# First unit of an attention and two-MLP kernel in two passes of 256 tokens, begun after two groups, on one core

## The reference, cut to what matters

```python
# attention: batch 4, heads 8, sequence 768, head size 48; y goes to x (3072 tokens x 384)
for t in range(S):
    cur = einsum('bhd,bhe->bhde', u * k_t, v_t)
    y[:, :, t] = einsum('bhd,bhde->bhe', r_t, state + cur)
    state = w_t[..., None] * state + einsum('bhd,bhe->bhde', k_t, v_t)
# first MLP, F1 = 768
h = maximum(maximum(x @ w1, x @ w2), x @ w3)
x = h @ w_out
# second MLP, F2 = 1024
h = x @ w_in;  e = exp(h - max(h));  sm = e / (sum(e) + 1e-9)
solu = h * sm
out = ((solu - mean) / sqrt(var + 1e-6) * g_ln) @ w_out2
```

## Time and profile before

| | |
|---|---|
| time, median of 3 runs (lowest, highest) | 776.88 us (776.53, 777.39) |
| the profiled execution: own time | 776.59 us |
| its span, first to last instruction | 774.8 us |
| TensorE busy (matmuls), weight loads | 727.5 us, 604.1 us |
| VectorE busy | 494.7 us |
| ScalarE, GpSimd busy | 296.4 us, 72.9 us |

### The profile page before, as it was taken

How to read it: one execution, slowest core, us unless ns; L and a number is a source line. 1 busy time by engine, 2 the same in 40 slices (tenths; PEclk the granted TensorE clock), 3 DMA queues, 4 the chain that set the end, 5 groups by cost and what they waited for, 6 DMA issues and landing times.

```text
span 774.8 us, 21949 instructions
## 1 busy us (share of the span) xinstructions
PE 727.5 (94%) x9280; PEld 604.1 (78%) x9280; DVE 494.7 (64%) x944; ACT 296.4 (38%) x698; POOL 72.9 (9%) x178
## 2 busy tenths in 40 slices
PE   4776999999999999999999999999999999999987
PEld 3666778778887778888878888877988877888776
DVE  5998666698455688566589566578665568222381
ACT  4434432674313445132447123336233236211260
POOL 2222301201011101011010011010110100000000
PEclk9956899999999999999999999999999999999999
DMA  7345523155222045420134511216611004400043
GB/s 243 114 129 172 178 87 107 32 152 177 89 79 78 5 126 178 128 78 20 60 109 148 178 51 43 64 42 186 186 45 40 2 7 135 130 10 1 1 136 121
DMA packets 56706, 74.92 MB, mean 97 GB/s; under 512 B 8224, under 2 KB 43296, under 8 KB 56608
## 3 DMA queue, kind: packets, MB, share of 16 engines
q1 hardware_dynamic: 56192, 73.44, 30.0%
q10 hardware_dynamic: 416, 0.08, 0.1%
HBM read 48.58 MB, written 22.54 MB: 92 GB/s over the span
## 4 chain that ended last, share of the span: by engine, by line
PE 78%; DVE 9%; issue 3%; DMA 3%; SPq 2%; ACT 1%; DVEq 0%; ACTq 0%
PE ps L608 17%; PE ps L609 15%; PE ps L610 15%; PE ps L667 14%; PE ps L564 10%; PE ps L585 3%; PE ps L603 3%; DVE z_blocks L869 2%; DVE rk_sb L804 2%; PE ps L594 1%; DMA z_turning<-z_blocks 1%; DMA zT<-z_turning 1%; DVE e_sb L909 1%; DVE neg_max L903 1%; DVE scoresT L825 1%
## 5 line engine op out<-in xcount | busy, mean ns | idle before, releaser
L667 PE MATMUL ps<-w_moe_out,zT 128*128 128x384 f32 x384 | 132.9, 499 | 8.5 <-ACT out_sb L782 4.8
L804 DVE TENSOR_TENSOR rk_sb<-rk_sb,decay 112x512 f32<-112x512 f32 x144 | 97.6, 698 | 54.4 <-PE ps L564 53.6
L608 PE MATMUL ps<-xT,w_moe 128*128 128x512 f32 x324 | 131.0, 404 | 0.3 <-issue 0.3
L667 PEld LDWEIGHTS ps<-w_moe_out,zT 128*128 128x128 f32 x384 | 118.5, 315 | 15.3 <-issue 6.0
L609 PE MATMUL ps<-xT,w_moe 128*128 128x512 f32 x324 | 126.9, 392 | 0.0
L610 PE MATMUL ps<-xT,w_moe 128*128 128x512 f32 x324 | 126.7, 391 | 0.0
L564 PEld LDWEIGHTS ps<-rk_sb 48*64 48x64 f32 x4224 | 86.0, 148 | 50.7 <-issue 34.2
L564 PE MATMUL ps<-rk_sb 48*64 48x32 f32 (+1 forms) x4224 | 98.2, 233 | 20.4 <-DVE rk_sb L804 16.9
L709 ACT COPY scoresT<-ps 16x128 f32<-16x128 f32 (+2 forms) x168 | 55.8, 333 | 87.5 <-PE ps L564 78.5
L752 ACT CAST h_x<-e_sb 128x512 fp32r<-128x512 f32 x36 | 22.4, 621 | 173.9 <-DVE e_sb L888 173.9
L832 DVE COPY_PREDICATED scoresT<-level_m,ps 64x256 f32<-64x256 uint32 x144 | 76.6, 532 | 4.0 <-PE ps L564 1.4
(11 more groups left out here) (78 smaller groups left out, 953.8 us busy)
## 6 DMA issues: line engine op xcount, KB each, us to landing
rk_sb<-in_rk SPq DMA_DIRECT2D x24, 512.0 KB, 4.2
z_turning<-z_blocks SPq DMA_DIRECT2D x24, 512.0 KB, 3.2
zT<-z_turning SPq DMA_DIRECT2D x96, 128.0 KB, 2.9
w_sb<-in_w SPq DMA_DIRECT2D x24, 224.0 KB, 4.0
k_turning<-k_blocks SPq DMA_DIRECT2D x20, 256.0 KB, 2.3
k_tok<-k_turning SPq DMA_DIRECT2D x80, 64.0 KB, 2.2
v_sb<-in_v SPq DMA_DIRECT2D x24, 192.0 KB, 4.2
out<-out_sb SPq DMA_DIRECT2D x24, 192.0 KB, 2.1
```

The source lines that it names most:

```text
L608: nc.tensor.matmul(o, a[0], b[0], start=first, stop=False)
L667: last = nc.tensor.matmul(ps[:, OUT, 0:DM], zT[:, t % 2, :, c], w_moe2_out[:, c, :], start=(c == 0), stop=(c == J2 - 1))
L804: nc.vector.tensor_tensor(both, both, by, ALU.mult).then_inc(scaled, 1)
```

## The change

- The `u` and `d` tasks of unit 0 are done in two passes of 256 tokens (`PASSES`, `tokens`), the first when groups 0 and 1 are done. Words `u`, `d` of the list are pass 0 and `U`, `D` pass 1 of that unit. Every `u` and `d` of both passes has as many matmuls as before, with 256 columns in place of 512. All other units are one pass.
- For groups 0 and 1 (`first`) VectorE masks all 128 tokens of a slot in one operation, on 128 partitions in place of twice 64. The late half's scores then lie in the columns of the early half, and `mix` makes y in two halves, with 24 matmuls on 64 rows of scores in place of 8, after which it needs no state product. The fourth pair of heads is written into its rows of `xT` by matmuls with `v_first` (a copy of v's pieces between zeros, a new DMA), so `y_last` and the six DMAs fall away for these two groups. GpSimd clears the part of `scoresT` afterwards; VectorE's memset at the start falls away.
- For groups 0 and 1 k is turned by four TensorE transposes into bank 7 with an identity (a new DMA on ScalarE's queue) and copied by ScalarE into `k_tok`, in place of VectorE's transpose and the two DMA steps.
- For groups 0 to 3 (`ZERO_GROUPS`) the state products are left out, since the state is zero, and ScalarE copies the update into `state` in place of VectorE's two operations.
- The four strings are written anew. In the new list the first `u` stands behind 22 slots (all of groups 0 and 1, five of group 2, one of group 3), two `M` and chunks 0 to 10. The second unit's first `u` stands in both lists behind the same work: all of unit 0, `M` 0 to 7, slots up to the sixth of group 8 and the second of group 9.

```diff
+PASSES = [B // 2, B // 2] + [B] * (UNITS - 1)
+P0 = [sum(PASSES[:n]) for n in range(len(PASSES) + 1)]
+ZERO_GROUPS = B
+FIRST_GROUPS = B // 2
...
-    v q 3 4 3 4 3 p b4 b5 4 z z M q p v z 4 a5"""
+    z 0 1 a2 0 1 0 z z z 1 z M q v 1 b2 2 2 1 2 z 2 z M a3 p v z q b3"""
...
+                if g < FIRST_GROUPS:
+                    if g == 0:
+                        pe.wait_ge(c_loaded, 16 * 3)
+                    else:
+                        pe.wait_ge(k_copied, g)
+                    for q in range(PAIRS):
+                        last = nc.tensor.transpose(ps[:, OUT, q * 128:(q + 1) * 128], k_sb[:, slot, q * C:(q + 1) * C], ident[:])
+                    last.then_inc(k_on_rows, 1)
+                if first(g):
+                    update()
+                    wait_y()
+                    wait_scores()
...
+                    for half in range(2):
+                        if half:
+                            pe.wait_ge(y_early, g + 1)
+                        rows, width = slice(half * HALF, (half + 1) * HALF), C - half * HALF
...
+            def up(n, j, w):
+                cols, i = tokens(n), 3 * j + w
+                if i == 0:
                     wait_split(3 * KD)
-                    pe.wait_ge(repacked, B * REPACK * (m + 1))
+                    if P0[n + 1] > FIRST_GROUPS:
+                        pe.wait_ge(repacked, REPACK * (P0[n + 1] - FIRST_GROUPS))
+                    else:
+                        pe.wait_ge(y_split, P0[n + 1])
...
                 for k in range(KD):
-                    last = product(ps[:, n % 2, :], [w_moe1[:, p, w * KD + k, j * 128:(j + 1) * 128] for p in range(2)],
-                                   [xT[:, p, k, :] for p in range(2)], k == 0, k == KD - 1)
+                    last = product(ps[:, i % 2, cols], [w_moe1[:, p, w * KD + k, j * 128:(j + 1) * 128] for p in range(2)],
+                                   [xT[:, p, k, cols] for p in range(2)], k == 0, k == KD - 1)
...
-                for h in range(2):
-                    rows = slice(h * HALF, (h + 1) * HALF)
+                for rows, at in ((slice(0, C), 0),) if first(g) else ((slice(0, HALF), 0), (slice(HALF, C), HALF)):
```

More of the change, by code:

```diff
@@ L13 @@
 TOK = B * C
+PASSES = [B // 2, B // 2] + [B] * (UNITS - 1)
+P0 = [sum(PASSES[:n]) for n in range(len(PASSES) + 1)]
+PASS_OF = [n for n, groups in enumerate(PASSES) for _ in range(groups)]
 DM = H * D
@@ L509, in _, with clears_before @@
             nc.gpsimd.memset(state[:], 0.0).then_inc(cleared, 1)
+            def clears_before(kind, n):
+                here = PROGRAM.index((kind, (n,)))
+                return 1 + sum(kind == "M" and FIRST_GROUPS - RING_P <= task[0] < FIRST_GROUPS for kind, task in PROGRAM[:here])
             def tree(g):
@@ L525, in split, with clear @@
                     return
+                pool.wait_ge(cleared, clears_before("z", c))
                 pool.wait_ge(w_hi, c + 1)
                 nc.gpsimd.tensor_tensor(chunk_of(c, 1), stage_of(c), chunk_of(c, 0).bitcast(f32), ALU.subtract).then_inc(w_split[1], 1)
-            run({"b": tree, "z": split})
+            def clear(g):
+                if FIRST_GROUPS - RING_P <= g < FIRST_GROUPS:
+                    here = PROGRAM.index(("M", (g,)))
+                    pool.wait_ge(tree_done, UPDATES * sum(kind == "b" for kind, _ in PROGRAM[:here]))
+                    chunks = sum(kind == "z" for kind, _ in PROGRAM[:here])
+                    if splits(chunks, True):
+                        pool.wait_ge(w_split[1], splits(chunks, True))
+                    pool.wait_ge(y_done, g + 1)
+                    nc.gpsimd.memset(scoresT[HB:128, g % RING_P, :, :, 0:HALF], 0.0).then_inc(cleared, 1)
+            run({"b": tree, "z": split, "M": clear})
         @block.tensor
@@ L570, in mix, with update @@
                 upd, yp = ps[:, LEV[1], :], ps[:, Y, :]
[L571 to L588, removed]
+                def update():
+                    if not 0 <= g - 1 < UPDATED_GROUPS:
+                        return
                     wait_drained(("upd", g - 1))
-                    pe.wait_ge(k_moved, 16 * BLOCKS * g)
+                    if g - 1 < FIRST_GROUPS:
+                        pe.wait_ge(k_copied, g)
+                    else:
+                        pe.wait_ge(k_moved, 16 * BLOCKS * (g - FIRST_GROUPS))
                     for q in range(PAIRS):
@@ new lines, in mix @@
+                if g == FIRST_GROUPS:
+                    pe.wait_ge(cleared, 1 + RING_P)
+                wait_y()
+                if g >= ZERO_GROUPS:
+                    signal, value = new_state_of(g - B)
+                    pe.wait_ge(signal, value)
+                for q in range(PAIRS if g >= ZERO_GROUPS else 0):
+                    cols = slice(q * C, (q + 1) * C)
+                    for i, rows in enumerate((HB, D)):
+                        part = slice(i * HB, i * HB + D)
+                        nc.tensor.matmul(yp[i * HB:i * HB + rows, cols], state[part, b, q, 0:rows], r_sb[part, slot, cols],
+                                         start=q == 0, stop=False, skip_group_check=True)
@@ L602, in mix @@
                     for i in range(2):
[L603 to L604 removed]
+                        rows = HB if g < ZERO_GROUPS and i == 0 else D
+                        at = (2 * q + i) * D
+                        last = nc.tensor.matmul(yp[i * HB:i * HB + rows, cols], v_sb[:, slot, at:at + rows],
+                                                scoresT[:, p, i, q, :], start=g < ZERO_GROUPS and q == 0, stop=True, skip_group_check=True)
                 last.then_inc(y_done, 1)
@@ L707, in scores @@
                     late = n * 2 * L + L
+                    if first(g) and L < HALF:
+                        late %= HALF
                     at = 0 if L == HALF else n * L % (HALF // 2)
@@ L783, in rows @@
                                      scale=row_scale[:, t:t + 1]).then_inc(out_ready, 1)
-            run({"a": base, "s": scores, "y": keep, "q": y_high, "u": up, "d": down, "e": exps, "c": centre, "w": rows, "z": split, "g": gain})
+            run({"a": base, "s": scores, "y": keep, "q": y_high, "u": up, "d": down, "e": exps, "c": centre, "w": rows, "z": split, "g": gain, "v": turned})
         @block.vector
         def _(dve):
-            nc.vector.memset(scoresT[HB:128, :, :, :, 0:HALF], 0.0).then_inc(cleared, 1)
-            dve.wait_ge(c_loaded, 16 * 2)
+            dve.wait_ge(c_loaded, 16 * 3)
             def scale(g, n):
```

249 lines of the change are left out of this document (163 added, 86 removed).

## The result

The changed kernel takes 772.63 us (771.64 to 773.65, 5 runs) beside 777.33 us (776.53 to 777.80) of the kernel before on the same chip: ratio 0.9941, 95% interval 0.9927 to 0.9956. It is 4.7 us faster; I had forecast 11.9. The span of its profiled execution is 769.6 us, 5.2 less than before.

What follows compares the result with a forecast made beforehand. TensorE was taken to bound all but the start, which VectorE sets. 44 + 121.7 + 11.1 + 3.0 + 4.8 + 6.0 put the second unit's first product at 190.6 us, 11.9 earlier: 764.7 us, range 755 to 776.

Steps and rivals of the forecast that it cites:

- TensorE bounds all but the start; an earlier start of the products pays.: Whole kernel: VectorE sets the start, TensorE the rest; first product from 80.75 to 44 us, time 11.9 us lower.
- Costs of what is moved: TensorE behind the first product: slots add 11.1 us, `M` 2 and 3 3.0, narrow `u` and `d` matmuls 4.8.
- my bounds of 0.114 and 0.189: Unit 0's 256-column matmuls: start distance between half of now, 0.114 us, and the recorded weight load, 0.189; 0.125 taken.
- my sum: Up to the second unit's first product: 44 + 121.7 + 11.1 + 3.0 + 4.8 + 6.0 = 190.6 us.
- Rival 1: Unit 0's narrow matmuls: weight loads bind at 0.189 us a start, 27.6 us more, 792 us; chance 0.09.
- First product at 44 us: Start-up: VectorE's 30.0 us of work from 9.15 gives 39.2, plus waits, 44 us; bounds 40 and 50.
- 3.5 + 1.5: VectorE's start-up: 3.5 us for slots closer to TensorE's latency, 1.5 us for the way through `M` 1 and copy.
- At 85% I take 6 to 7% of 90 us.: First product to first `l`: VectorE 85% busy, so TensorE stalls 6 us more; bounds 2 and 15.
- the checkpoint: The second unit's first product, forecast at 190.6 us, 11.9 earlier than the 202.46 of before.
- rivals 2 (771 to 776): First unit: VectorE binds, stalls 15 us, first product at 46, gain 1 to 5 us; chance 0.17, 0.04 for worse.
- 3 (771): Start-up: the early start doesn't come, first product at 50 us as chunk loads wait, gain 6 us; chance 0.08.
- Later units near 120 us, nothing won or lost: Steady and last units: new orders taken as 0, with 3 us either way; steady units still near 120 us.

Runs made afterwards that it cites:

- e7: Changed kernel's groups 0 to 3, but unit 0 in one pass of 512 columns with START and FIRST of before; 779.54 us, ratio 1.0024.
- e1: Changed kernel with the lone slots of unit 0's second MLP put in pairs again; 765.25 us, ratio 0.9844 to the kernel before.
- e2: Changed kernel with 14 matmuls that nobody reads put behind the second slot of group 8, filling the first wait; 769.36 us, ratio 0.9893.

## Why the prediction was right in kind and wrong in size

- *TensorE bounds all but the start; an earlier start of the products pays.* Right: e7 without the early start is no faster than before, e1 with it is 12.1 us faster by its ratio (0.0156 x 776.6).
- *Costs of what is moved.* Slots 11.1 as forecast, `M` 3.1 for 3.0, `u` and `d` 5.2 for 4.8. Two products of 256 columns start 0.120 us apart, between my bounds of 0.114 and 0.189. The changed kernel, TensorE:

```profile
47.55 0.41 PE L716 MATMUL ps<-xT,w_moe 128*128 128x256 f32 x1
47.77 0.41 PE L717 MATMUL ps<-xT,w_moe 128*128 128x256 f32 x1
...
53.33 0.28 PE L716 MATMUL ps<-xT,w_moe 128*128 128x256 f32 x1
53.45 0.28 PE L717 MATMUL ps<-xT,w_moe 128*128 128x256 f32 x1
```

  I took 0.125, so the stream is 2 us cheaper than in my sum; the first 16 or so, 0.214 apart, and the first matmul behind each slot cost that and 0.4 more. Rival 1, weight loads that bind, is refuted. The Trainium skill, "TensorE: Matmul & The Clock Gate", section "Back-to-back issue gap", gives 262 cycles for 256 columns, 0.109 us at 2.4 GHz; the trace has 0.120, with a weight load in front of each.
- *First product at 44 us.* It came at 46.75, 2.75 late. The masks on 128 partitions do cost what I took, 0.42 (`base_m`) and 0.43 or 0.73 us (predicated), and VectorE's work is 29.1 us for my 30.0. What failed is the waiting: VectorE idles 8.8 us between its first mask and the first product, where my sum has 3.5 + 1.5. I summed VectorE's queue and put the lengthening of TensorE's `M` 0 and 1 at nothing: they last some 5 and 6 us at the slow pace, where 3.75 and 4.6 stood before, 2.7 us more together. That this is what makes the 2.75 us is an argument from these lengths; no run shortens the two `M` alone.
- *"At 85% I take 6 to 7% of 90 us."* This step failed. In the stretch I named, VectorE was busy 69.6 us (80%) for my 76, and TensorE idled 1.1 us, 0.2 more than before. The other 4.2 us of extra idle time came in the next stretch, which I had left as it was, because I read VectorE's share and not the order: I weighed the new orders of the steady and last units, and not that of unit 0's second MLP. There, two places where two slots stand apart with no TensorE work between cost 5.5 us of waits. In e1, with as much for VectorE to do, the idle time up to the checkpoint is only 0.4 us above that of before. So 4.4 us for my 6.0 is luck and no confirmation.
- *The clock.* My sum has no term for it. The two `o` behind the waits are 3.8 us longer together; e2 shows that idleness does it, e1 that both go when the slots stand in pairs. e1's checkpoint, 187.95 us, lies 8.5 us ahead of the changed kernel's and 2.7 ahead of my 190.6: 5.5 of waits and 3.8 of clock, less what the remaining waits take.
- *What makes the gain at the checkpoint 5.8 us smaller than forecast.* First product 2.75, `o` 3.8, `u` and `d` 0.4, `l` 0.3 and `M` 0.1 more than in my sum, idle time 1.6 less. The time, 772.63 us, lies where rivals 2 (771 to 776) and 3 (771) put theirs, but by neither mechanism: the additional idle time was 4.4 and not 15 us, and the first product did come early.
- *Later units near 120 us, nothing won or lost.* 120.08 for 120.17; 0.9 us is lost behind the checkpoint, all of it in the fifth unit's second MLP (from its first `l` to the last unit's first product), 47.85 for 46.94 us. e2 has the same lists there and takes 46.97, so this may be a difference between executions and no price of the change; it was not tried.

## What to carry to other kernels

Where a list fixes the order on all engines, read what stands between two uses of the same buffer on the engine that bounds: if only other engines' tasks stand there, look for a wait, whatever the busy shares say; here VectorE was 67% busy in the stretch with both waits. Price a wait on TensorE with what follows it as well: here the matmuls behind waits of 2.2 and 3.3 us took 1.7 to 2.5 us longer. Work taken from a busy engine in a start-up phase is worth only what the steps and the pace of the other engines leave (e7: 9.2 us less on VectorE, nothing won), and a run with that part alone tells it at once. The version to keep is e1, 765.25 us, faster than both kernels.

## What the runs showed of the hardware

In the changed kernel's first 46.75 us the granted clock reads 1.00, but the first products of 256 columns start 0.214 us apart, which is 1.2 GHz, and a few us later 0.120. Slots show the same: 0.67 us for 32 records in the dense stream, 1.08 at the start. So the record of the clock there does not tell the pace; the distance of starts does. The kernel before ran some slots of its start at 0.67 us, e7 almost none. And 2.2 to 3.3 us of idleness in a dense stretch were followed by an `o` of 7.2 to 8.06 us in place of 5.55, while behind a wait of 1.11 us in the kernel before `o` took 5.55.
